# Inner units of an expert network renumbered, two loads swapped at the start, and a table read into registers at another place

## The reference

```python
# layer 1: taps
w = softmax(weight_gen, axis=-1)                  # [2, 3584, 8 heads, 7]
out = einsum('bshk,bskhg->bshg', w, x_unfolded)   # 24 columns per head
# layer 2: two choices of 8 experts
noisy = x @ w_gate + log1p(exp(x @ w_noise)) * noise
top2 = the two largest of noisy;  top2_w = softmax of the two
for e in range(8):
    h = np.maximum(x[mask] @ w1[e], 0.0)          # [., 1024] inner units
    out[mask] += top2_w[mask, k, None] * (h @ w2[e])
# layer 3: one choice of 8 experts
expert_idx = argmax(x @ w_gate);  gate_w = softmax(x @ w_gate)[expert_idx]
for e in range(8):
    out[mask] = gate_w[mask, None] * (np.maximum(xe @ w1[e], 0.0) @ w2[e])
```

## Time and profile before

| | us |
|---|---|
| median of 3 runs | 1132.88 (1132.68 to 1135.5) |
| the profiled execution, its own time | 1142.65 |
| its span, first to last instruction | 1140.9 |

### The profile page before, as it was taken

How to read it: one execution, slowest core, us unless ns; L and a number is a source line. 1 busy time by engine, 2 the same in 40 slices (tenths; PEclk the granted TensorE clock), 3 DMA queues, 4 the chain that set the end, 5 groups by cost and what they waited for, 6 DMA issues and landing times.

```text
span 1140.9 us, 30614 instructions
## 1 busy us (share of the span) xinstructions
PE 1081.1 (95%) x7894; PEld 1009.4 (88%) x7895; DVE 796.5 (70%) x1432; ACT 571.5 (50%) x1233; POOL 488.9 (43%) x530
## 2 busy tenths in 40 slices
PE   3999899999999999999999999999999899999995
PEld 2779699898999899999999899998888888999995
DVE  8996899998588754456566775556668874656652
ACT  2345145455544344445566344445765654555542
POOL 1000255656444444444445344454445544544452
PEclk9997799998999999999999999999999999999998
DMA  8439133333323242454554332335964634543510
GB/s 254 128 101 290 36 98 112 116 100 106 103 77 95 82 112 85 126 154 146 173 166 126 102 97 90 94 110 172 273 188 143 159 106 115 157 126 111 150 46 14
DMA packets 105111, 143.77 MB, mean 126 GB/s; under 512 B 27818, under 2 KB 82413, under 8 KB 104812
## 3 DMA queue, kind: packets, MB, share of 16 engines
q1 hardware_dynamic: 85612, 99.74, 30.4%
q0 software_dynamic: 19456, 43.53, 13.3%
HBM read 111.53 MB, written 35.09 MB: 129 GB/s over the span
## 4 chain that ended last, share of the span: by engine, by line
PE 69%; DVE 12%; issue 8%; DMA 4%; ACT 2%; DVEq 2%; SPq 1%; POOL 1%; ACTq 1%; POOLq 0%
PE ps_y L1903 17%; PE ps_y L1909 8%; PE ps_h L1840 7%; PE ps_h L1844 6%; PE ps_h L1847 6%; PE ps_h L1841 5%; PE ps_h L1828 4%; PE ps_h L1660 3%; DVE h_lo L1084 2%; PE ps_y L1930 2%; DVE prod L957 2%; PE ps_x L1818 2%; PE ps_x L1817 2%; DMA row<-in_moe_w_dram 1%; PE ps_y L1936 1%
## 5 line engine op out<-in xcount | busy, mean ns | idle before, releaser
L1903 PE MATMUL ps_y<-w_hl,h_hi 128*128 128x400 f32 (+1 forms) x1344 | 370.9, 360 | 3.1 <-DVE y L1104 1.5
L1084 DVE SCALAR_TENSOR_TENSOR h_lo<-ps_h,h_hi 128x512 fp32r<-128x512 f32 x404 | 258.7, 686 | 155.8 <-ACT h_hi L1502 117.3
L597 POOL DMA_INDIRECT row<-x_rows,read_now x200 | 229.9, 1149 | 287.5 <-issue 243.7
L1502 ACT ACTIVATE h_hi<-ps_h 128x512 fp32r<-128x512 f32 x370 | 202.7, 596 | 227.1 <-PE ps_h L1828 142.6
L1909 PE MATMUL ps_y<-w_hl,h_lo 128*128 128x200 f32 (+1 forms) x1344 | 293.9, 259 | 2.8 <-DVE h_lo L1084 2.7
L1903 PEld LDWEIGHTS ps_y<-w_hl,h_hi 128*128 128x128 f32 x1344 | 244.6, 188 | 4.4 <-issue 2.6
L1909 PEld LDWEIGHTS ps_y<-w_hl,h_lo 128*128 128x128 f32 x1344 | 235.6, 191 | 4.8 <-DVE h_lo L1084 4.8
L1840 PE MATMUL ps_h<-xa_hi,w1a_hi 128*128 128x256 f32 x672 | 203.7, 303 | 5.0 <-ACT xa_hi L1431 3.1
L1844 PE MATMUL ps_h<-xa_lo,w1a_hi 128*128 128x256 f32 x672 | 192.0, 286 | 3.4 <-DVE xa_lo L1066 3.4
L1841 PE MATMUL ps_h<-xa_hi,w1a_lo 128*128 128x256 f32 x672 | 190.1, 283 | 0.0
L1847 PE MATMUL ps_h<-xb_hh,w1b_hl 128*128 128x256 f32 x672 | 189.3, 282 | 0.0
(11 more groups left out here) (245 smaller groups left out, 1652.0 us busy)
## 6 DMA issues: line engine op xcount, KB each, us to landing
w_raw<-in_moe_w_dram SPq DMA_DIRECT2D x32, 768.0 KB
w1a_raw<-in_moe_w_dram SPq DMA_DIRECT2D x32, 512.0 KB
w1b_raw<-in_moe_w_dram SPq DMA_DIRECT2D x64, 256.0 KB
x_rows<-tok SPq DMA_DIRECT2D x14, 512.0 KB, 3.3
x_rows<-tok SPq DMA_DIRECT2D x28, 256.0 KB
x_pad<-in_x_dram SPq DMA_DIRECT2D x2, 2688.0 KB, 10.6
row<-x_rows,read_now POOLq DMA_INDIRECT x200
x_pad<-y_rows SPq DMA_DIRECT2D x14, 200.0 KB
```

Of the source, the lines that this page charges most:

```text
L597: pool.indirect_dma_start(out=row[:, buffer, u, 0:XW if p < C else SCALED_W], out_offset=None, in_=x_rows[p], in_offset=bass.IndirectOffse ...
L1084: nc.vector.scalar_tensor_tensor(out=h_lo[:, i * GF:(i + 1) * GF, :], in0=ps_h[:, i, :].rearrange("p (f t) -> p f t", f=GF), scalar=0.0, i ...
L1502: act.activation(h_hi[:, i * GF:(i + 1) * GF, :], ps_h[:, i, :].rearrange("p (f t) -> p f t", f=GF), ACT.Relu).then_inc(h_hi_ready, 1)
L1903: nc.tensor.matmul(first, h_hi[:, i, cols], both_w, start=(i == 0), stop=False)
```

## The change

It has four parts.

1. The inner units are numbered otherwise: chunk c holds the units m*8 + c for m from 0 to 127. So partition p holds rows 8p to 8p+7 of `w2`, 6144 bytes that lie together in DRAM (`load_w2`, `stage_w2`). The layout of `w2` in SBUF and all products stay as they are.
2. `w1` is loaded as before. The splits of `w1` on ACT and DVE, which used to read it with step 1, now read it through `by_chunk` with a step of 8 elements (32 bytes); what they write keeps its layout.
3. SP issues `load_chunk(1)` ahead of the four loads of expert 1's weights.
4. DVE reads the bounds of pass 0 into registers between the reciprocals and the first multiplication of `softmax_divide(1, ...)`. The wait for the softmax's last step moves from the end of that function to the start of `convolution` and of `experts(0)`.

```diff
+        softmax_done = [sem(f"softmax{c}_done") for c in range(C)]
...
+        def by_chunk(raw):
+
+            return raw[:, :].rearrange("p (m c) -> p c m", c=FC)
...
             def load_w2(layer, e):
                 w2 = LAYER_W[layer][1]
-                sp.dma_start(w2_raw[:, :, :], w2[e, :, :].rearrange("o (c p) d -> p (o c) d", p=P)).then_inc(w2_loaded, 16)
+                sp.dma_start(w2_raw[:, :, :], w2[e, :, :].rearrange("o (p c) d -> p (o c) d", p=P)).then_inc(w2_loaded, 16)
...
             def stage_w2(e):
 
-                w2 = LAYER_W[0][1][e:e + 1, :, :].rearrange("o (c p) d -> p (o c) d", p=P)
+                w2 = LAYER_W[0][1][e:e + 1, :, :].rearrange("o (p c) d -> p (o c) d", p=P)
...
             stage_w2(E - 1)
+            sp.wait_ge(w2_turned_ps, E - 1)
+            load_chunk(1)
             sp.wait_ge(w_lo_ready, 3)
             load_w1a(0, slice(1, 2))
             load_w1b(0, slice(1, 2))
             load_w2(0, slice(1, 2))
-            sp.wait_ge(w2_turned_ps, E - 1)
-            load_chunk(1)
...
                     nc.vector.reciprocal(tap_stat[:, h], tap_stat[:, h]).then_inc(done, 1)
+                if ahead is not None:
+                    ahead()
...
-                dve.wait_ge(done, 8)
...
+                dve.wait_ge(softmax_done[c], 8)
                 dve.wait_ge(x_loaded, 48 * (c + 1))
...
# DVE, split_w1a
-                nc.vector.tensor_tensor(lo, w1a_raw[:, :], hi.bitcast(F32), ALU.subtract).then_inc(w_lo_ready, 1)
+                nc.vector.tensor_tensor(lo, by_chunk(w1a_raw), hi.bitcast(F32), ALU.subtract).then_inc(w_lo_ready, 1)
...
# DVE, split_w1b
-                raw = w1b_raw[:, :].rearrange("p (c a m) -> p c a m", a=2, m=P)
+                raw = w1b_raw[:, :].rearrange("p (m c a) -> p c a m", a=2, m=P)
...
-                g0 = first_tile(dve, p)
+                if p == 0:
+                    g0, (last0, n, _) = first_bounds
+                    dve.wait_ge(softmax_done[1], 8)
+                else:
+                    g0 = first_tile(dve, p)
+                    last0, n, _ = tile_bounds(dve, p, E - 1)
...
+            def load_first_bounds():
+
+                dve.wait_ge(routed, 1)
+                first_bounds.append(first_tile(dve, 0))
+                first_bounds.append(tile_bounds(dve, 0, E - 1))
+
+            softmax_divide(1, softmax_done[1], load_first_bounds, lambda: split_rows(0))
...
# ACT, split_w1a and split_w1b
-                act.activation(w1a_hi_both[:, bass.ds(b, 1), :].rearrange("p o f -> p (o f)"), w1a_raw[:, :], ACT.Copy).then_inc(w_hi_ready, 1)
+                act.activation(w1a_hi_both[:, bass.ds(b, 1), :].rearrange("p o (c m) -> p (o c) m", m=P), by_chunk(w1a_raw), ACT.Copy).then_inc(w_hi_ready, 1)
...
-                act.activation(w1b_hl_both[:, bass.ds(b, 1), :].rearrange("p o f -> p (o f)"), w1b_raw[:, :], ACT.Copy).then_inc(w_hi_ready, 1)
+                act.activation(w1b_hl_both[:, bass.ds(b, 1), :].rearrange("p o (c m) -> p (o c) m", m=P), by_chunk(w1b_raw), ACT.Copy).then_inc(w_hi_ready, 1)
```

More of the change, by code:

```diff
@@ L695, in softmax_shift, with softmax_divide @@
                                             ALU.subtract).then_inc(taps_shifted, 1)
-            def softmax_divide(c, between=None):
-                done = sem(f"softmax{c}_done")
+            def softmax_divide(c, done, ahead=None, between=None):
                 for i, h in enumerate(TOKEN_HALVES):
@@ L1010, in split_w1a @@
             def split_w1a(s, b):
-                hi, lo = (buf[:, bass.ds(b, 1), :].rearrange("p o f -> p (o f)") for buf in (w1a_hi_both, w1a_lo_both))
+                hi, lo = (buf[:, bass.ds(b, 1), :].rearrange("p o (c m) -> p (o c) m", m=P) for buf in (w1a_hi_both, w1a_lo_both))
                 dve.wait_ge(w_hi_ready, 3 * s + 1)
-                nc.vector.tensor_tensor(lo, w1a_raw[:, :], hi.bitcast(F32), ALU.subtract).then_inc(w_lo_ready, 1)
+                nc.vector.tensor_tensor(lo, by_chunk(w1a_raw), hi.bitcast(F32), ALU.subtract).then_inc(w_lo_ready, 1)
             def split_w1b(s, b):
                 hl = w1b_hl_both[:, bass.ds(b, 1), :].rearrange("p o (c a m) -> p (o c) a m", a=2, m=P)
-                raw = w1b_raw[:, :].rearrange("p (c a m) -> p c a m", a=2, m=P)
+                raw = w1b_raw[:, :].rearrange("p (m c a) -> p c a m", a=2, m=P)
                 dve.wait_ge(w_hi_ready, 3 * s + 2)
@@ L1168, in experts @@
                 nonlocal g2
-                g0 = first_tile(dve, p)
+                if p == 0:
[4 more added lines that the diff above has]
+                    last0, n, _ = tile_bounds(dve, p, E - 1)
                 if p == C:
                     g2 = dve.snap(g0)
-                last0, n, _ = tile_bounds(dve, p, E - 1)
                 if p == 3:
@@ L1219, in _ @@
             softmax_shift(0)
-            softmax_divide(0)
+            softmax_divide(0, softmax_done[0])
             convolution(0, range(NB))
@@ L1241, in _ @@
             list_rows(0)
-            softmax_divide(1, lambda: split_rows(0))
+            first_bounds = []
+            def load_first_bounds():
[3 more added lines that the diff above has]
+            softmax_divide(1, softmax_done[1], load_first_bounds, lambda: split_rows(0))
             for p in range(PASSES):
```

## The result

The changed kernel takes 1173.02 us (median of 4 runs, 1167.15 to 1175.53) where the kernel before, on the same chip, takes 1134.19 (median of 4, 1132.68 to 1135.83). The ratio is 1.031, 95% interval 1.027 to 1.035: slower by 38.8 us. The forecast was slower by 10.6 us with 1157.0 as the upper end of its range. So the direction held and the size did not. The profiled execution took 1171.37 us, its span is 1169.6; that of the kernel before, 1142.65 us, was a long one, so the two traces are only 28.7 us apart.

A forecast was written before the change was run, and what follows sets the result against it. The prediction took PE as the bound, with DVE equally busy in the first stretch. Its terms, +5.5 +7 +0.5 -1.4 -1.0 = +10.6 us on the 1132.88 us median, gave about 1143.5 us, range 1130.5 to 1157.

The forecast's parts named there:

- Bound: Over the tiles: DVE and PE both busy in the first stretch, PE alone later; DVE can make PE wait at xa_lo.
- Price per element: In the w1 splits on DVE and ACT: 0.82 ns more per element at 32-byte step, 0.84 us per split.
- The scan's row: Routing scans of 28 floats at 32-byte step, 208 ns against 185 for neighbours; source of the 0.82 ns upper bound.
- First stretch, +5.5: From 137 to 292 us, eight longer DVE splits ahead of xa_lo: +5.5 us, bounds 0 and 6.7.
- The other tiles, +7: Later tiles, 54 split steps exceeding the room at xa_lo: +7 us; bounds 0 and 16, at 0.3 us per step.
- Before the tiles, +0.5: Expert 0's longer splits in and behind the first layer: +0.5 us, bounds 0 and 1.7.
- Table, -1.4: Table loads moved behind the softmax's reciprocals, before DVE's first product: -1.4 us, bounds -0.8 and -2.0.
- `w2` in one piece, -1.0: ACT's 7 waits for w2 loads, 7.0 us, shrink and perhaps a third reaches PE: -1.0 us, bounds 0 and -2.9.
- Order of loads, 0: At the start, expert 1's loads go out some 12 us later but land before the first tile: 0 us.
- The free step: Rival: DVE and ACT read at 32-byte step at full rate, leaving parts 1 and 4: 1130.5 us; chance 0.15.
- the cheap one: Rival: 0.4 us per split, felt in the first stretch and pass 2: 1135 to 1137 us; chance 0.14.
- The dear step: Rival: 1.7 us per split, first stretch 13 us, later steps about 0.7 over their room: about 1180 us; chance 0.07.

The follow-up runs named there:

- the kernel with pairs: Against the kernel before, both engines' w1a splits and ACT's w1b copies read neighbouring pairs with a 64-byte hop; up to tile 66, 1.0 us ahead of before.
- the operation at step 2: One of seven unused DVE operations added to the kernel before: a 512-element subtraction with one source at step 2; 0.60 us against 0.58 for neighbours.
- DVE alone: Against the kernel before, only DVE's w1 splits read with a step of 8 elements; timed with w2 loaded in one piece: 1162.9 us, ratio 1.023.
- ACT alone: Against the kernel before, only ACT's copies of w1a and w1b read with a step of 8 elements: 1155.4 us, ratio 1.016.
- the kernels with short splits: Six kernels, the one before included, whose w1 splits stay short; about 164.6, 490.5 and 321.1 us for tiles 0 to 15, 15 to 66, 66 to 99.
- the piece alone: Against the kernel before, only w2's loads changed, to one piece per partition: 1121.9 us, ratio 0.987, with one tile fewer in layer 3.

## Why the prediction was right or wrong, point by point

**Bound: right.** PE sets the pace, DVE too in the first stretch, and `xa_lo` is where a longer split shows.

**Price per element: right for DVE, short for ACT, and from a row that didn't hold it.** 0.84 us per split was forecast; `split_w1a` grew by 0.96, the two halves by 0.93 together, ACT's copies by 1.17 and 1.20. The scan's row came near by chance. It also gave an upper bound, 0.82 ns, that was none: ACT is another engine, and 28 elements were too few to bound 1024. The Trainium skill's page Vector Engine (DVE) Microarchitecture Reference, section "Measured stream behaviour on trn2", gives rates from which the prediction estimated 0.7 us for 1024 elements, nearer to DVE's value than a free step but below it. Its rule that the full rate needs adjacent pairs fits the kernel with pairs and not the operation at step 2, which kept the rate without pairs: the measurement decides. The Trainium skill's page SBUF — State Buffer, section "Door 1: The DMA port swizzle", says that two accesses are needed per 16-byte line; this agrees with all steps of DVE here (2 free, 4 and 8 not, pairs free), while the "4 fp32" that the Trainium skill gives there as a free stride does not (0.98 against 0.58 us).

**First stretch, +5.5: DVE's part right, ACT's missing.** DVE alone cost 6 to 7 us up to tile 15. ACT added 3, to 10. The forecast had charged ACT's copies nothing here, though ACT's `w1a` copy stands between the second and the third `h_hi`.

**The other tiles, +7: this is the step that failed.** Measured, it is about 10 us to tile 66 and 13 behind it, 23 for the change. The forecast took 0.1 us on average for a step, because there were 0.6 us of room at `xa_lo` and DVE needed 0.84. It let ACT "eat some room" and gave that no number. In fact ACT's longer copy comes first (DVE's wait 0.21 to 2.02 us) and DVE's longer split behind it, so that `xa_lo` ended 0.79 us after the first product of tile 45 where it had ended 0.38 us before it. With ACT alone it ended 0.7 to 0.8 us after it, with DVE alone 0.25 us before it. That is a mis-sized term through an unpriced path, as ACT alone at +19 us shows. The upper bound, 16, was made of 0.3 us per step and so didn't contain it.

**What is left over.** The columns of the table give 10 + 10 + 13 = 33 us for the change against the kernels with short splits. The other 6 of the 38.8 us can't be placed by these traces.

**A wait that the forecast didn't name.** PE's first product waits 6.8 us for `split_w1b` in layer 3.

**Before the tiles, +0.5:** no effect that can be told from the clock's. DVE's part was covered by the 7.6 us wait, which is still 7.6.

**Table, -1.4: right where the copies are short (1.6 us), and nothing in the change,** for what is late next was not DVE's own stretch but ACT's copy of `w1a` in the first tile.

**`w2` in one piece, -1.0: not shown.** ACT's wait for it went from 7.0 us to 1.7 with the piece alone, and PE did not gain. That it is 0 in the change says little, since with ACT alone stepping and the old pieces it is 0.2 or less. The lower bound of the term, -2.9, was given without a working. **Order of loads, 0:** nothing in the traces speaks against it; it wasn't tried apart from the table.

**The rivals.** The free step and the cheap one (0.4 us per split) fall with the durations of the splits, 0.93 to 1.20 us more. The dear step had the time (about 1180) and the wrong reason: its price was 1.7 us per split, nearly twice the measured one on DVE, while the excess that it put in, 0.7 us per step, is near what the tile above shows: PE's third product stood 0.26 us behind the tile's first, and now 0.85. It took no more than ACT's 1.2 us to make nearly all of it (0.75 to 0.82 us with ACT alone), not 1.7 of DVE.

## What to carry to other kernels

If an edit makes several engines slower, follow each one's extra time through the whole tile to the place where they meet, and price each alone and both together, since here they added up in some tiles and not in others: a copy on an engine that is half idle can stand ahead of what the busy one waits for. The price of an access pattern is taken from an operation of the same kind at about the same length, else its bounds are wider than the rows suggest. And an experiment that changes values may change the routing: count the instructions before comparing times.

## What the runs showed of the hardware

- Reading 4-byte elements at a step of 8 bytes is free on VectorE (0.60 against 0.58 us for 512, and 688 against 686 ns with all three operands stepping) and costs ScalarE 0.09 us in 1.06. At 16 bytes VectorE pays 0.78 ns per element, at 32 bytes 0.78 to 0.93; ScalarE pays 1.15 at 32.
- Pairs of elements with a hop of 64 bytes are free on VectorE (1215 ns) and nearly so on ScalarE (1122 against 1061).
- A weight load of TensorE with a step of 32 bytes takes 339 ns instead of 190 for 128 columns, and the kernel in which TensorE reads `w1` so takes 1.334 times as long.
- A scan over 28 elements takes as long over neighbours (0.22 us) as at a step of 32 bytes (0.21).
